# Turning the router's rows by DMA transposes instead of through PE in a fused attention and mixture-of-experts kernel

## The chip, the cores and the metric

The kernel runs on one core of one Trainium2 chip. The metric is the device time of the whole kernel in microseconds (us). Smaller is better. The core has five engines that run their own instruction streams and meet only at semaphores: PE (matrix products and transposes into PSUM), DVE, ACT and POOL (elementwise work), and SP, which here only issues DMAs.

## The reference

Two things are computed one after the other, for 2 batches of 768 positions:

```python
# attention with hash buckets, 16 heads (2 batches x 8) of 64 columns
scores = np.where(q_bucket == k_bucket, scale * q @ k.T, -1e9)
attn   = softmax(scores)
x      = attn @ v                       # (2, 768, 512), float32
# router
logits     = x @ w_gate                 # 8 experts
local_gate = sigmoid(x @ w_local)       # under 0.5: the fresh expert, else that of the position before
# experts, two layers with relu, one expert per position
out[s] = p[e] * (max(x[s] @ w1[e], 0) @ w2[e])
```

The router needs x transposed: the product over the 512 model columns wants those columns on the partitions.

## The kernel before

**Constants.** P = 128 partitions, NH = 16 heads, J = 6 row blocks of a batch, NC = 12 row blocks in all, DC = 4 column blocks of 128, NS = 48 attention steps (three per head: n = 3h + p). LEAD = 5 and LAG = 2 are how far scores run ahead and values behind.

**Attention.** Step n of PE's loop makes the transposed scores of step n (`scores_t`, L640 and L641), other preparation, and the values product of step n - 2 (`values`, L673 to L684). ACT takes exponentials (`exps`, L757) and their high half-precision part (`high`, L763). POOL subtracts to get the low part (`low`, L547); for the last two steps DVE does (`low_last`, L875). DVE normalises a finished head (`norm`, L881 to L891) and so writes two half-precision parts, high and low, of the head's 64 columns of x into XNS. Heads 0 to 7 are batch 0, heads 8 to 15 batch 1. A head's 64 columns are half a column block, so column block 3 of batch 1 is heads 14 and 15. Each engine's order is written out by hand: what stands earlier in an engine's loop runs earlier, and an instruction that waits holds all behind it on that engine.

**The router's rows.** For each of the 12 row blocks, `turn_rows` makes 8 PE transposes of 128 x 128 (two parts times four column blocks, L305) into a PSUM buffer `pG`, `copy_rows` copies the 128 x 1024 block to SBUF (`XTC`, L324 on DVE, L322 on ACT), and `logits` makes 12 small matmuls with 9 output columns (L313). Row blocks are numbered i. The six of batch 0 go i = 0 to 3 in steps 44 to 47 of the attention, i = 4 and 5 between and behind the last values. The six of batch 1, i = 6 to 11, come behind the last head (`rows_done(pe, NH - 1)`). ACT copies i = 4, 6, 8, 10, each behind half a piece of weight work; DVE the others.

**Behind the logits.** DVE waits for `s_gl` (all 12 row blocks) and for `s_rc` (small constants that POOL makes) and then runs a serial chain with PE that assigns positions to 19 tiles of 128 slots. It ends in the slot table (L1192 to L1194). POOL then gathers x rows by tile with indirect DMAs (`gather`, L1302), interleaved with the low parts of expert weights (`low_weights`, L407). ACT makes full scale and high parts of weights (`scale_weights`, L391; `high_weights`, L397; later L1446 and L1457) and issues weight loads (L1260). PE runs, per tile, `up` (24 matmuls, L1364; L1390 for the first tile) and `down` (24 matmuls, L1405). SP turns the gathered rows and the hidden rows with DMA transposes of 128 x 1024 half-precision elements (`turn_x`, L1276; `turn_h`, L1283).

**Queues.** SP issues in order: the max row of head 15 (`place_row`, L433) in step 43, then nothing until step 50, where it waits for the last head and issues the six x row stores of batch 1 (L518), two weight loads (L416), and, once `s_gl` and the stores have landed, eight quarter loads (L1260). POOL makes the small constants (L1042 to L1059) as soon as the last head is normalised, then `low_weights(6)`. The room in SBUF is shared by hand: XTC lay over the buffers T1 and T2; the four operand buffers OPS begin at CHUNK.

Of the kernel before, what the change touches and what calls it, by code (L numbers as in the profile page):

```python
# [6 lines left out]
def lsh_attention_moe_kernel(nc, q, k, v, proj, w_gate, w_local, w1, w2, x_rows, w_parts, out):  # L7
# [55 lines left out]
    with ctx:  # L63
# [67 lines left out]
        XTC = room[:, T_AT:T_AT + 3 * DM].bitcast(f16).rearrange("p (i a n) -> p i a n", i=3, a=2)  # L131
# [114 lines left out]
        s_wgp = sem("s_wgp")  # L246
        s_gt = sem("s_gt")
        s_gha = sem("s_gha")
        s_gc = sem("s_gc")
# [27 lines left out]
        pG = [o.bitcast(f16).rearrange("p (a n) -> p a n", a=2) for o in (pA[:, 0:512], pA[:, 512:1024], pB[:, 0:512])]  # L277
        pL = pA[:, 1024:1536]

        def logits_of(i):  # L280


            half = NC // 2
            if i < half:
                return i * B, i % 2, i - 1
            return (i - half) * B + 1, i % 3, i - 1 if i < half + 2 else 0 if i == half + 2 else i - 2

        def by_act(i):

            return i >= NS - TAIL and i % 2 == 0  # L290

        def copied(eng, i):

            if by_act(i):
                eng.wait_ge(s_gha, sum(by_act(k) for k in range(i + 1)))
            else:
                eng.wait_ge(s_gc, sum(not by_act(k) for k in range(i + 1)))

        def turn_rows(pe, i):
            c, buf, before = logits_of(i)  # L300
            if before > 0:
                copied(pe, before - 1)
            for a in range(2):
                for d in range(DC):
                    last = pe.transpose(pG[buf][:, a, d * P:(d + 1) * P], XNS[:, c, a, d * P:(d + 1) * P], idh[:, :])  # L305
            last.then_inc(s_gt, 1)

        def logits(pe, i):
            c, buf, _ = logits_of(i)
            copied(pe, i)  # L310
            for d in range(DC):
                for m, (a, r) in enumerate(((0, WGL), (1, WGH), (0, WGH))):
                    last = pe.matmul(pL[:, c * (E + 1):(c + 1) * (E + 1)], XTC[:, buf, a, d * P:(d + 1) * P], r[:, d, :],  # L313
                                     start=d == m == 0, stop=d == DC - 1 and m == 2)
            last.then_inc(s_gl, 1)

        def copy_rows(eng, i):
            _, buf, before = logits_of(i)
            eng.wait_ge(s_gt, i + 1)
            wait(eng, s_gl, before)  # L320
            if by_act(i):
                eng.activation(XTC[:, buf, :, :], pG[buf], ACT.Copy).then_inc(s_gha, 1)  # L322
            else:
                eng.tensor_copy(XTC[:, buf, :, :], pG[buf]).then_inc(s_gc, 1)  # L324


        TAIL = NS - LEAD + 1
# [124 lines left out]
        def _(sp):  # L452
# [118 lines left out]
        def _(pe):  # L571
# [133 lines left out]
            for n, h, p in steps():  # L705
# [14 lines left out]
                i = n - TAIL  # L720
                if pair(n - LAG) and n < NS:
                    values(n - LAG)
                    if 0 < i:
                        logits(pe, i - 1)
                    if 0 <= i:
                        if i == 0:
                            pe.wait_ge(s_wgp, 2)
                            pe.wait_ge(s_rmax, NS)
                            rows_done(pe, NH // B - 1)
                        turn_rows(pe, i)  # L730
                if p == 0 and fresh(h + 3):
                    turn_qk(h + 3, 0)

            values(NS - 2)
            turn_rows(pe, NS - TAIL)
            values(NS - 1)
            for i in range(NS - TAIL, NC // 2):
                logits(pe, i - 1)
                if i + 1 < NC // 2:
                    turn_rows(pe, i + 1)  # L740
# [791 lines left out]
```

## Time and profile before

| what | us |
|---|---|
| median of 3 runs | 486.23 |
| lowest and highest | 483.11, 488.06 |
| the profiled execution | 485.34 |
| its span on the core | 483.5 |
| PE busy | 455.8 |
| POOL busy | 340.0 |
| ACT busy | 302.1 |
| DVE busy | 262.5 |
| mean granted TensorE clock | 0.987 |

A time in the trace is counted from the start of the span. Busy is the sum of an engine's instructions. PE's matmuls are pipelined, so a busy PE is not yet one that nothing could make faster; the chain of work that ended last tells more. Between the span and the profiled execution's time lie 1.8 us.

### The profile page before, as it was taken

Reading aid. Unit: us, or ns where it says so; the run is one execution under the profiler, and the core shown is the slowest. Engines: PE = TensorE matmul, PEld = TensorE weight load, DVE = VectorE, ACT = ScalarE, POOL = GpSimd, SP = SyncE. Lnnn points to the kernel's source line nnn. Section 1 sums busy time; section 2 is a strip of 40 time slices with the busy share of each in tenths; the row PEclk is TensorE's granted clock in tenths of the full one; section 3 lists DMA queues with packets and bytes.
Section 4 is the critical chain, followed back from the end, with each engine's and each line's share of the span. In section 5 each row is a group of like instructions: output and inputs, shape, how many; then the busy total and the mean of one; then the engine's idle time right before and its main releaser. Section 6 shows DMA issues by size and latency. Waiting matters only on the chain.

```text
span 483.5 us, 11076 instructions
## 1 busy us (share of the span) xinstructions
PE 455.8 (94%) x4238; PEld 269.3 (56%) x4238; DVE 262.5 (54%) x385; ACT 302.1 (62%) x284; POOL 340.0 (70%) x193
## 2 busy tenths in 40 slices
PE   6699999999998999999977899999999999899994
PEld 3356777777666776767765344444444444344441
DVE  5676677666665666665475855344443344316331
ACT  2348988878888898887868145876566557600000
POOL 1226889897988798999824499999795847961101
PEclk9989999999999999999998899999999999999998
DMA  7745754566545833224009699999999999763440
GB/s 187 179 106 132 195 101 135 157 173 167 147 108 135 269 88 86 53 56 175 3 6 354 206 205 271 260 266 283 250 249 280 241 247 257 154 180 83 92 64 1
DMA packets 145284, 79.80 MB, mean 165 GB/s; under 512 B 90627, under 2 KB 136079, under 8 KB 145234
## 3 DMA queue, kind: packets, MB, share of 16 engines
q1 hardware_dynamic: 97726, 40.03, 38.1%
q10 hardware_dynamic: 44468, 30.93, 25.3%
q0 software_dynamic: 3040, 8.13, 5.5%
q8 instruction: 37, 0.61, 0.5%
q14 instruction: 13, 0.11, 0.1%
HBM read 47.99 MB, written 8.13 MB: 116 GB/s over the span
## 4 chain that ended last, share of the span: by engine, by line
PE 58%; ACT 13%; POOL 9%; ACTq 7%; DMA 4%; issue 3%; DVE 3%; SPq 1%; DVEq 0%
ACTq L1260 7%; ACT W L1457 7%; PE pA L623 6%; PE pB L641 6%; PE pA L624 6%; PE pB L640 6%; POOL W L407 6%; PE pO L1405 4%; PE pO L684 3%; PE pO L679 3%; PE pO L681 3%; PE pA L1364 3%; PE pP L1405 3%; POOL room L1302 3%; ACT room L1446 3%
## 5 line engine op out<-in xcount | busy, mean ns | idle before, releaser
L547 POOL TENSOR_TENSOR room<-room 128x1536 f16<-128x1536 f32 x46 | 142.5, 3106 | 39.0 <-ACT room L763 38.9
L407 POOL TENSOR_TENSOR W<-room,W 128x1024 f16<-128x1024 f32 x48 | 100.7, 2111 | 13.9 <-ACT W L1457 11.7
L854 DVE TENSOR_REDUCE room<-pA 128x2 f32<-128x1536 f32 x46 | 80.9, 1758 | 51.7 <-PE pA L624 51.7
L757 ACT ACTIVATE room<-pB 128x1536 f32<-128x1536 f32 x48 | 69.5, 1449 | 37.4 <-PE pB L641 36.1
L763 ACT ACTIVATE room<-room 128x1536 f16<-128x1536 f32 x48 | 71.2, 1484 | 1.5
L679 PE MATMUL pO<-W,room 128*128 128x64 f16 x576 | 62.0, 192 | 0.0
L684 PE MATMUL pO<-W,room 128*128 128x65 f16 x576 | 62.0, 194 | 0.0
L681 PE MATMUL pO<-W,room 128*128 128x65 f16 x576 | 61.9, 193 | 0.0
L640 PE MATMUL pB<-room 128*128 128x512 f16 x192 | 57.8, 326 | 0.4 <-ACT room L757 0.4
L641 PE MATMUL pB<-room 78*128 78x512 f16 x192 | 57.9, 326 | 0.0
L623 PE MATMUL pA<-room 128*128 128x512 f16 (+1 forms) x184 | 55.4, 326 | 1.5 <-DMA room<-room 1.4
L624 PE MATMUL pA<-room 76*128 76x512 f16 (+1 forms) x184 | 55.5, 326 | 0.0
L679 PEld LDWEIGHTS pO<-W,room 128*128 128x128 f16 x576 | 53.0, 98 | 2.3 <-issue 0.2
L681 PEld LDWEIGHTS pO<-W,room 128*128 128x128 f16 x576 | 52.9, 97 | 2.2
L1405 PE MATMUL pO<-W,room 128*128 x240 | 53.4, 379 | 0.0
L684 PEld LDWEIGHTS pO<-W,room 128*128 128x128 f16 x576 | 52.6, 97 | 0.0
L1309 POOL DMA_INDIRECT out<-room x19 | 18.9, 993 | 43.3 <-DVE room L1485 40.1
L1364 PE MATMUL pA<-W,room 128*128 x216 | 48.1, 379 | 1.3 <-POOL W L407 1.3
L1364 PE MATMUL pB<-W,room 128*128 x216 | 48.1, 379 | 0.6 <-DMA room<-room 0.6
L1405 PE MATMUL pP<-W,room 128*128 x216 | 48.1, 379 | 0.0
L1405 PEld LDWEIGHTS pO<-W,room 128*128 128x128 f16 x240 | 23.5, 98 | 28.3
L407 POOL TENSOR_TENSOR W<-XN,W 128x1024 f16<-128x1024 f32 x16 | 33.7, 2135 | 6.6 <-ACT W L1457 6.6
(219 smaller groups left out, 781.7 us busy)
## 6 DMA issues: line engine op xcount, KB each, us to landing
room<-in_moe_w ACTq DMA_DIRECT2D x44, 256.0 KB
room<-room SPq DMA_DIRECT2D x93, 96.0 KB, 2.2
W<-in_moe_w ACTq DMA_DIRECT2D x8, 1024.0 KB, 5.9
XN<-in_moe_w ACTq DMA_DIRECT2D x28, 256.0 KB
W<-in_moe_w SPq DMA_DIRECT2D x4, 1024.0 KB, 7.1
room<-in_q SPq DMA_DIRECT2D x16, 192.0 KB, 3.5
W<-in_v ACTq DMA_DIRECT2D x4, 768.0 KB, 6.3
x_rows<-XN SPq DMA_DIRECT2D x12, 256.0 KB, 3.2
```

What stands on the lines that cost most here:

```text
L407: pool.tensor_tensor(parts(r)[:, 1, cols], scaled(r)[:, cols], parts(r)[:, 0, cols], ALU.subtract).then_inc(lows(r, half)[0], 1)
L547: pool.tensor_tensor(PTL[:, n % NP, :, :], E32[:, n % 2, :, :], PTH[:, n % NP, :, :], ALU.subtract).then_inc(s_lo, 1)
L623: pe.matmul(o, QA[:, b, cols], KA[:, b, n0:n1], start=True, stop=False)
L624: last = pe.matmul(o, QB[0:R_S, b, cols], KB[0:R_S, b, n0:n1], start=False, stop=True)
L640: pe.matmul(o, KA[:, b, cols], QA[:, b, n0:n1], start=True, stop=False)
L641: last = pe.matmul(o, KB[0:R_ST, b, cols], QB[0:R_ST, b, n0:n1], start=False, stop=True)
L679: pe.matmul(o, PTH[:, n % NP, i, cols], VL[g // HG][:, g % HG, j, :], start=False, stop=False, skip_group_check=True)
L681: pe.matmul(o1, PTL[:, n % NP, i, cols], VH[g // HG][:, g % HG, j, 0:D + 1], start=False, stop=False, skip_group_check=True)
L684: last = pe.matmul(o1, PTH[:, n % NP, i, cols], VH[g // HG][:, g % HG, j, 0:D + 1], start=False, stop=j == J - 1, skip_group_check=True)
L854: dve.reduce_max(RM[:, g % 2, 2 * p:2 * p + 2], scores_in(n)[:, :].rearrange("p (i s) -> p i s", i=2), AX.X).then_inc(s_rmax, 1)
L1364: last = pe.matmul(o, l[:, cols], r, start=k == m == 0, stop=k == n - 1 and m == 2)
L1405: last = pe.matmul(pY[t % 2][:, 0:DM], HT[:, t % 2, a, f * P:(f + 1) * P], W[:, bass.ds(at + low * CHUNK, 512)], start=a == f == 0 and low ...
```

## The change

The six row blocks of batch 0 are turned by six DMA transposes of 128 x 1024 elements each, issued by SP in step 43, into a buffer of their own. Column blocks 0 to 2 of batch 1 are turned by twelve DMA transposes of 128 x 384 elements (six row blocks, two parts), issued by SP in step 45. PE makes the logits of batch 0 two row blocks at a time in steps 46 and 47 and the last two behind the last values, then the part of batch 1's logits that comes from column blocks 0 to 2. Behind the last head only column block 3 of batch 1 goes through PE: 12 transposes in two groups of six, one copy of 128 x 768 on DVE, one on ACT, and 18 matmuls. ACT does all four pieces of weight 6 first and the copy after them. POOL does `low_weights(6)` ahead of the small constants instead of behind them. ACT's first half of `scale_weights(7)` moves behind the exponential of the logits.

```diff
+        XTC = [room[:, at:at + J * DM].bitcast(f16).rearrange("p (i a n) -> p i a n", i=J, a=2) for at in (CHUNK, T_AT)]
...
+        pG = [pA[:, k * 512:(k + 1) * 512].bitcast(f16)[:, 0:J * P] for k in range(2)]
...
+        def logits(pe, b, i, blocks):
+            c = i * B + b
+            for d in blocks:
                 for m, (a, r) in enumerate(((0, WGL), (1, WGH), (0, WGH))):
+                    last = pe.matmul(pL[:, c * (E + 1):(c + 1) * (E + 1)], XTC[b][:, i, a, d * P:(d + 1) * P], r[:, d, :],
+                                     start=c == d == m == 0, stop=d == DC - 1 and m == 2, skip_group_check=True)
+            return last
+        TURNS = (NS - LEAD, NS - LEAD + 2)
...
+                if n == TURNS[0]:
+                    sp.wait_ge(s_ST, PAIRS * (NH - 2))
+                    sp.wait_ge(s_PV, PAIRS * (NH - 3) + 1)
+                    rows_done(sp, H - 1)
+                    for i in range(J):
+                        sp.dma_start_transpose(XTC[0][:, i, :, :].rearrange("p a (d n) -> p (a d) n", n=P),
+                                               XNS[:, i * B, :, :].rearrange("p a n -> p (a n)")).then_inc(s_xt_in[0], 16)
+                if n == TURNS[1]:
+                    sp.wait_ge(s_qkt, 2 * NH)
+                    sp.wait_ge(s_hash, 2 * NH)
+                    for g in (NH - 2, NH - 1):
+                        sp.wait_ge(s_asm[g % NQ], 96 * (g // NQ + 1))
+                    rows_done(sp, NH - 3)
+                    for i in range(J):
+                        for a in range(2):
+                            sp.dma_start_transpose(
+                                XTC[1][:, i, a, 0:(DC - 1) * P].rearrange("p (d n) -> p d n", n=P),
+                                XNS[:, i * B + 1, a, 0:(DC - 1) * P]).then_inc(s_xt_in[1], 16)
...
                 if pair(n - LAG) and n < NS:
                     values(n - LAG)
-                    if 0 < i:
-                        logits(pe, i - 1)
-                    if 0 <= i:
...
-                        turn_rows(pe, i)
+                i = B * (n - TURNS[0] - 3)
+                if 0 <= i < J and n < NS:
+                    if i == 0:
+                        pe.wait_ge(s_wgp, 2)
+                        pe.wait_ge(s_rmax, NS)
+                        rows_turned(pe, 0)
+                    for k in range(i, i + B):
+                        logits(pe, 0, k, range(DC)).then_inc(s_gl, 1)
...
             values(NS - 2)
-            turn_rows(pe, NS - TAIL)
             values(NS - 1)
...
+            for k in range(B * (NS - TURNS[0] - 3), J):
+                logits(pe, 0, k, range(DC)).then_inc(s_gl, 1)
+            rows_turned(pe, 1)
+            for i in range(J):
+                logits(pe, 1, i, range(DC - 1))
+            rows_done(pe, NH - 1)
+            for k in range(2):
+                for i in range(HJ):
+                    for a in range(2):
+                        at = (2 * i + a) * P
+                        last = pe.transpose(pG[k][:, at:at + P], XNS[:, (k * HJ + i) * B + 1, a, (DC - 1) * P:DC * P], idh[:, :])
+                last.then_inc(s_gt, 1)
+            for k in range(2):
+                pe.wait_ge(s_gc[k], 1)
+                for i in range(k * HJ, (k + 1) * HJ):
+                    logits(pe, 1, i, range(DC - 1, DC)).then_inc(s_gl, 1)
...
             norm(NH - 1)
-            for i in range(NS - TAIL, NC // 2):
-                if not by_act(i):
-                    copy_rows(dve, i)
+            dve.wait_ge(s_gt, 1)
+            dve.tensor_copy(last_rows_in(0), pG[0].rearrange("p (k n) -> p k n", n=P)).then_inc(s_gc[0], 1)
...
         def _(pool):
+            low_weights(pool, EARLY, 0)
+            low_weights(pool, EARLY, 1)
             pool.wait_ge(s_x, NH)
...
-            low_weights(pool, EARLY, 0)
-            low_weights(pool, EARLY, 1)
...
             for piece in (scale_weights, high_weights):
                 for half in range(2):
                     piece(act, EARLY, half)
-                    copy_rows(act, next(rows))
+            act.wait_ge(s_gt, 2)
+            act.activation(last_rows_in(1), pG[1].rearrange("p (k n) -> p k n", n=P), ACT.Copy).then_inc(s_gc[1], 1)
+            act.wait_ge(s_dl, 1)
+            act.activation(EX[:, :, :], DL[:, :, :], ACT.Exp, scale=1.0 / (XS * WS)).then_inc(s_ex, 1)
             act.wait_ge(s_PV, NS - LAG)
             scale_weights(act, EARLY + 1, 0)
...
         def _(pe):
-            rows_done(pe, NH - 1)
-            for i in range(NC // 2, NC):
-                turn_rows(pe, i)
-                if i > NC // 2 + 1:
-                    logits(pe, i - 2)
-            logits(pe, NC - 2)
-            logits(pe, NC - 1)
```

## Rows read from the trace of the kernel before

**Rows 1.** The chain in order of time: start us, us, what.

```profile
260.10 0.27 DVE room L1138
...
271.26 1.15 POOL room L1302
...
410.12 4.24 POOL W L407 x2
414.49 5.35 PE pA L1364 x24
```

**Rows 2.** Stretches: us, busy us of PE, PEld, DVE, ACT, POOL, granted clock, DMA share, GB/s.

```profile
260.00:272.00 12.00, 9.65 (x64) 4.22 (x63) 10.08 (x50) 7.25 (x9) 1.46 (x2) 0.72 0.85 315
283.00:414.00 131.00, 129.72 (x600) 58.64 (x600) 61.30 (x56) 87.82 (x88) 109.56 (x62) 1.00 1.23 260
```

**Rows 3.** PE's longest waits from 270 on: us in total, times, longest.

```profile
PE pA L1364 <- POOL W L407: 1.3, 1, 1.3
```

**Rows 4.** DVE's timeline: start us, us, engine, line, form [idle before <-releaser].

```profile
247.46 1.76 DVE L875 TENSOR_TENSOR room<-room 128x1536 f16<-128x1536 f32 x1 [0.62 <-ACT room L763]
250.64 0.17 DVE L881 TENSOR_SCALAR DEN<-pO 128x6 f32<-128x6 f32 x1 [0.82 <-PE pO L684]
252.26 0.56 DVE L891 TENSOR_TENSOR XN<-pO,XN 128x384 f16<-128x384 f32 x1
258.33 0.69 DVE L324 COPY room<-pB 128x1024 f16<-128x1024 f16 x1 [1.17 <-PE pB L305]
```

**Rows 5.** PE's timeline around step 47 and behind the last head.

```profile
242.95 0.38 PE L640 MATMUL pB<-room 128*128 128x512 f16 x1
254.68 0.61 PE L305 MATMUL pB<-idh,XN 128*128 128x128 f16 x8
265.66 4.53 PE L1091 MATMUL pP<-W,idh 128*128 128x512 f16 x12
```

**Rows 6.** PE's logits in the chain that ended last: start us, us, what.

```profile
259.23 0.77 PE pA L313 x24
```

**Rows 7.** ACT's timeline.

```profile
244.47 1.45 ACT L757 ACTIVATE room<-pB 128x1536 f32<-128x1536 f32 x1 [0.19 <-PE pB L641]
247.34 1.04 ACT L391 ACTIVATE room<-W 128x1024 f32<-128x1024 f32 x1
258.15 1.02 ACT L322 ACTIVATE room<-pA 128x1024 f16<-128x1024 f16 x1
262.26 2.00 ACT L397 ACTIVATE W<-room 128x1024 f16<-128x1024 f32 x2
```

**Rows 8.** POOL's timeline.

```profile
252.91 0.20 POOL L1042 TENSOR_SCALAR room<-col_id 128x8 f32<-128x8 f32 x1 [8.59 <-DVE XN L891]
253.78 0.10 POOL L1052 MEMSET room<- 128x2 f32 x1
256.49 4.23 POOL L407 TENSOR_TENSOR W<-room,W 128x1024 f16<-128x1024 f32 x2 [1.81 <-ACT W L397]
```

**Rows 9.** SP's issues, timeline: start us, us, what (a group with several: their sum).

```profile
231.89 1.41 SPq L433 DMA_DIRECT2D room<-room  x2
252.90 3.24 SPq L518 DMA_DIRECT2D x_rows<-XN  x6
276.61 7.22 SPq L1276 DMA_TRANSPOSE room<-room  x3
419.92 1.23 SPq L1276 DMA_TRANSPOSE room<-room  x1
456.20 2.61 SPq L1283 DMA_TRANSPOSE room<-XN  x2
```

**Rows 10.** DMA from 419 to 424 us, 40 slices of 0.125: busy tenths, GB/s.

```profile
DMA  0000000000000000189999999982000000000000
GB/s 0 0 0 0 0 0 0 0 0 0 0 0 0 0 0 0 23 172 231 211 221 213 209 197 215 203 167 37 0 0 0 0 0 0 0 0 0 0 0 0
```

**Rows 11.** Busy by stretch over the last steps of attention, columns as in rows 2.

```profile
233.40:242.80 9.40, 8.93 (x188) 7.35 (x187) 2.91 (x7) 8.16 (x7) 8.13 (x4) 1.00 0.02 4
```

More of the change, by code:

```diff
@@ L246, in lsh_attention_moe_kernel @@
         s_wgp = sem("s_wgp")
+        s_xt_in = [sem(f"s_xt_in{b}") for b in range(B)]
         s_gt = sem("s_gt")
-        s_gha = sem("s_gha")
-        s_gc = sem("s_gc")
+        s_gc = [sem(f"s_gc{k}") for k in range(2)]
         s_gl = sem("s_gl")
@@ L275, in prep_in @@
             return pO if g < AHEAD and half == 1 else pP
-        pG = [o.bitcast(f16).rearrange("p (a n) -> p a n", a=2) for o in (pA[:, 0:512], pA[:, 512:1024], pB[:, 0:512])]
+        pG = [pA[:, k * 512:(k + 1) * 512].bitcast(f16)[:, 0:J * P] for k in range(2)]
         pL = pA[:, 1024:1536]
[L280 to L311, printed above, removed]
-                for m, (a, r) in enumerate(((0, WGL), (1, WGH), (0, WGH))):
[L313 to L324, printed above, removed]
@@ L329, in lsh_attention_moe_kernel, with last_rows_in @@
+        def last_rows_in(k):
+            return XTC[1][:, k * HJ:(k + 1) * HJ, :, (DC - 1) * P:DC * P].rearrange("p i a n -> p (i a) n")
+        TURNS = (NS - LEAD, NS - LEAD + 2)
         LAST = NS - 2
@@ L937, in _ @@
                     low_last(n)
-                i = n - TAIL
-                if 0 <= i < NS - TAIL:
-                    if i == 0:
-                        dve.wait_ge(s_asm[(NH - 1) % NQ], 96 * ((NH - 1) // NQ + 1))
-                        dve.wait_ge(s_asm[(NH - 2) % NQ], 96 * ((NH - 2) // NQ + 1))
-                    copy_rows(dve, i)
             norm(NH - 1)
-            for i in range(NS - TAIL, NC // 2):
-                if not by_act(i):
-                    copy_rows(dve, i)
+            dve.wait_ge(s_gt, 1)
+            dve.tensor_copy(last_rows_in(0), pG[0].rearrange("p (k n) -> p k n", n=P)).then_inc(s_gc[0], 1)
         pS, pR = pO, pB[:, 512:1024]
@@ L1060, in _ @@
                       allow_small_or_imprecise_dtypes=True).then_inc(s_rc, 1)
-            low_weights(pool, EARLY, 0)
-            low_weights(pool, EARLY, 1)
         @block.scalar
         def _(act):
-            rows = filter(by_act, range(NC))
             for piece in (scale_weights, high_weights):
@@ L1127, in _ @@
             ch = Chain(dve, s_rt)
-            for i in range(NC // 2, NC):
-                if not by_act(i):
-                    copy_rows(dve, i)
             dve.wait_ge(s_rc, 9)
```

15 lines of the change are left out of this document (2 added, 13 removed).

## The prediction, made before the changed kernel ran

> **What bounds the kernel now.** I read the chain that ended last first, in order of time. Through the router it is one serial thread: PE's logits, DVE's first reduction at 260.10 and, 11.16 us later, POOL's first gather at 271.26 [rows 1]. From there POOL, ACT and the load issues carry it to 410, and PE alone to the end. The stretches say more: from 283 to 414 PE is busy for 129.7 of 131 us [rows 2], and its longest wait for weights after 270 is 1.3 us [rows 3]. So behind 271 two streams are both nearly full, PE and POOL with ACT. Both start from the same slot table. If the table comes earlier, both start earlier, and the end moves with them. If one of them had a fixed start, the end would not move. I see none: the weight loads that fill the DMA engines are issued by ACT behind POOL's work.
>
> Then I read the timelines of each engine from 230 to 272. Behind the last head (norm(15) ends at 252.82) DVE waits another 7.3 us for the logits [rows 1, 4]. PE, DVE and ACT pass six row blocks of batch 1 round: 8 transposes, a copy of 0.69 or 1.02 us, 12 matmuls [rows 4, 5, 7]. ACT is the slow member, since a weight piece of 1.0 us stands between its copies. Over the last steps of attention the DMA engines are idle: share 0.02 from 233.4 to 242.8 [rows 11].
>
> **What goes.** 84 of 96 PE transposes, 10 of 12 large copies, and six trips PE, copy, PE behind the last head.
>
> **What comes on SP, batch 0.** SP is free after the max row of head 15, at 231.89 + 1.41 = 233.3 [rows 9]; the semaphores it then waits for belong to step 41 and are long there. One DMA transpose of 128 x 1024 takes 1.23 us to issue, two in a row 2.61, so 1.31 each [rows 9]. Issued alone at 419.92, its data moves from 421.0 to 422.5 at 200 to 215 GB/s [rows 10], so it has landed about 2.55 us after its start. The sixth starts at 233.4 + 5 x 1.31 = 239.95 and lands at 242.5.
>
> PE wants them in step 46, before scores_t(47), which began at 242.95 [rows 5]. Ahead of it now stand 24 logits: 0.77 us [rows 6], 0.6 without the tail that overlaps. So 242.35 is the landing at which nothing is lost. What is queued behind this wait is scores_t(47), then exps(47) at 244.47 [rows 7], low_last(47) at 247.46 and values(47), which ends at 250.64 [rows 4]: all of it sets the end of attention. Against that, steps 44 and 45 lose a turn of 8 transposes ahead of each scores_t, 0.45 us that comes back if the rows have landed. Bounds: attention ends 0.6 us earlier (rows landed) to 0.5 later (1.37 us an issue). I take 0.3 later, since the landing is what PE meets last: norm(15) ends at 253.1.
>
> Here a rule of the Trainium skill can be weighed. The row shows 200 to 215 GB/s for a transpose that is alone [rows 10]. The Trainium skill, Advanced Engine Details and Errata, section X-Bar Transpose (TRN2), says that transpose DMAs are as fast as regular ones, 350 to 400 GB/s. By that the sixth would land some 0.6 us earlier and PE would not wait; the trace does not agree, and I go by the trace.
>
> **Batch 1, column blocks 0 to 2.** SP starts them at 233.4 + 6 x 1.31 = 241.2. No row shows a 128 x 384 transpose. Lower bound: three eighths of 1.23, 0.46. Upper bound: the full 1.27. Plain issues cost 3.24 / 6 = 0.54 whatever they carry [rows 9]; taking 0.4 to 0.54 as fixed and three eighths of the rest gives 0.71 to 0.80. I take 0.77: issues end at 250.4, landing about 1.0 later at 251.4. PE asks at 250.9 + 0.6 for the last two blocks of batch 0, so 251.5: hidden, by attention itself. The 54 matmuls take 54 x 0.026 = 1.4 us, to 252.9, still before norm(15). SP reaches the x stores before the last head is done, so nothing queued behind (stores, weight loads) is late.
>
> **Behind the last head.** Transposes from 253.1: 8 take 0.61 with their tail [rows 5], six 0.5, twelve 0.8. DVE's copy of 128 x 768: 0.55; ACT's 0.8, from 253.9 to 254.75, both three quarters of the variable part of the large copies [rows 4, 7]. Nine matmuls 0.35. Logits complete: **255.1**.
>
> **The POOL move.** DVE also waits for nine small constants. Before, they took 252.91 to 253.88, hidden [rows 8]. Now low_weights(6) stands ahead. ACT starts weight 6 at 247.34 + 0.3 = 247.65, four pieces at 1.0 [rows 7]; the first high half is done at 250.7. POOL: 250.75 + 4.23 = 255.0, constants 0.97 [rows 8]: **256.0**. So the constants and not the logits release DVE, 0.9 us after them. What is moved past is nothing that anyone waited for; without the cover of the logits the move costs this 0.9. Bounds 255.7 to 256.5.
>
> **The router's serial part** stays 11.16 us. It contains 12 idle matmuls of PE in 4.53 us at a granted clock of mostly half (0.72 over the stretch) [rows 2, 5]. At half throughout (1.2 GHz) they would take 12 x 0.43 = 5.1. PE has less work ahead of them now. I add 0.2, bounds 0 to 0.6. The first gather meets the tail of weight loads, which still run to about 270: 0.1, bounds 0 to 0.8.
>
> **Sum.** 260.10 - 256.0 = 4.1 earlier, less 0.2 and 0.1: 3.8. Against the profiled execution (485.34; span 483.5 and 1.8 around it) 481.5; against the median shown, 486.23, which is 0.9 above it, **482.4**. With the bounds together the gain is 2.2 to 5.1: 481.1 to 484.0 on the median. The single runs of before spread by 2.5 us either way, so I widen this case's own range to 479.5 to 485.
>
> **Rivals.**
> - A: the small transposes cost as much to issue as the large. SP ends at 241.2 + 12 x 1.27 = 256.4, landing 257.4, PE's 54 matmuls 258.8, then 2.0: 260.8, 0.7 later than before. The stores start 3.5 us later and the loads behind them meet the gathers: 0.5. **487.4**. For it: nothing shows that the cost follows size; plain DMAs don't. Against: 1.23 beside 0.54 says that most of it follows blocks. It starts to cost at 0.87 each and eats the gain at 1.21. Chance 0.13.
> - B, the other side: six in a row back up, as three did at 276.61 in 7.22 us, 2.4 each [rows 9]. The sixth lands at 233.4 + 12 + 2.55 = 248.0, 5.6 past the point that costs nothing; PE stands in step 46 with scores_t(47) behind it. At half of that for each small one, SP ends at 262.2, logits at 262.2 + 1.0 + 1.4 + 2.0 = 266.6, 6.5 later: **492.7**. It decides from 1.86 us an issue. Against: those three stood among gathers, while here the DMA share is 0.02 [rows 11]. Chance 0.1.
> - C: the table is earlier, but PE or the weight stream is held by something else, and most of the gain comes back as PE waits before 414: **485.5**. Against: PE's 1.3 us of waiting says that the streams are balanced, for: balanced streams leave little to hide a shift in one. Chance 0.1.
> - D: batch 0's rows are there when PE asks; attention ends 0.6 earlier instead of 0.3 later: **481.5**. Chance 0.08. The rule of the Trainium skill named above would bring this about; the trace's rate speaks against it.
> - E: the clock stays at its lower level through all idle matmuls and the gathers lose 0.8 to the loads: 1.1 less gain, **483.5**. Chance 0.04.
> - The forecast: 0.55.
>
> **How the numbers follow.** 1% either way, about what can be told from no change, is 481.4 and 491.1. The forecast lies 0.8% below, so its better side is over the line: about 0.25 for faster, with D. Slower is B and a bad form of A, 0.12. The rest, 0.63, within 1%. The range takes in the forecast, D, E, C and A: 479.5 to 488; outside are B and what is better than all sums.
>
> **What would show it.** SP: six transposes from 233.3 to about 241.2, twelve to about 250.4; over 252.8 means A. PE: a wait in step 46 for a DMA of 0.1 to 1 us; over 3 means B. DVE's wait for the first reduction ends by POOL's constants, at 256.0. First gather near 267.5. From 283 on PE is as full as before; waits for POOL or a DMA there over 3 us mean C. I am wrong in kind if the rows' path still ends later than 258, or if the gather moves by over 3 us and the end does not.

## The result, and the profile after

The changed kernel is slower, by 1.3%. It took 492.99 us, the median of 4 runs (489.37 to 496.86), against 485.36 us for the kernel before, the median of 4 (483.11 to 488.06): a ratio of 1.0127, 95% interval 1.0068 to 1.0187. The prediction was 482.4 us, 0.8% faster. Here and below a ratio compares undisturbed executions alone, and one more than 1.5% above the fastest of its kernel is left out of it, while medians and means over all runs take in every execution. The profiled execution of the changed kernel took 489.37 us, its span is 487.6 us.

The attention's last heads don't start at the same time in any two traces: the first DVE instruction of norm(13), long before any changed instruction matters, lies at 232.46 in the trace of before and at 227.34 in this one, and a second trace of the kernel before has it at 228.06. So I call that instruction the mark and count from it.

| us behind the mark | before | after | forecast |
|---|---|---|---|
| SP has issued batch 0's six transposes | – | 10.04 | 8.7 |
| SP has issued batch 1's twelve | – | 27.4 | 17.9 |
| last head normalised (norm(15) ends) | 20.36 | 24.82 | 20.6 |
| first reduction on the logits | 27.64 | 32.85 | 23.5 |
| first gather starts | 38.79 | 44.12 | 35.0 |

The slot table, on which everything behind depends, comes 5.3 us later instead of 3.8 us earlier. First SP's issues in the changed kernel (start us, us, queue, line, form), which answer to [rows 9]:

```profile
226.77 1.41 SPq L407 DMA_DIRECT2D room<-room  x2
228.29 9.09 SPq L481 DMA_TRANSPOSE room<-XN  x6
237.62 17.11 SPq L492 DMA_TRANSPOSE room<-XN  x12
254.83 3.28 SPq L512 DMA_DIRECT2D x_rows<-XN  x6
```

The six large ones take 9.09 / 6 = 1.52 us each. The twelve, each with three eighths of the data, take 17.11 / 12 = 1.43 each. The same two groups once more, now with the shortest, median and longest issue in ns, and with the time from issue to landing:

```profile
L481 SPq DMA_TRANSPOSE room<-XN x6: 1329/1356/1998, 228.3 to 235.9; - x6
DMA to landing us min/median/max: 3.4/4.2/5.0
L492 SPq DMA_TRANSPOSE room<-XN x12: 1248/1257/2161, 237.6 to 253.5; - x12
DMA to landing us min/median/max: 2.3/2.4/4.4
```

Then PE's timeline (start us, us, line, form [idle before <-releaser]), to be read beside [rows 5]:

```profile
240.40 0.17 PE L292 MATMUL pA<-WGL,room 128*128 128x9 f16 x1 [3.71 <-DMA room<-XN]
...
241.03 0.59 PE L634 MATMUL pB<-room 128*128 128x512 f16 x1
...
243.12 0.63 PE L635 MATMUL pB<-room 78*128 78x512 f16 x1
...
255.88 0.19 PE L292 MATMUL pA<-WGL,room 128*128 128x9 f16 x1 [5.35 <-DMA room<-XN]
```

PE stands twice, 3.71 us in step 46 for batch 0's rows and 5.35 us for batch 1's, with 24 and 54 small matmuls behind. Between them stands something that I had not priced: the same 128 x 512 matmul of scores_t(47) that took 0.38 us before [rows 5] takes 0.59 here. The stretches say why. Columns as in [rows 2]: the granted clock, the DMA share and GB/s are the last three.

```profile
239.00:240.00 1.00, 0.00 (x0) 0.00 (x0) 1.00 (x1) 0.00 (x0) 0.00 (x0) 0.54 0.97 213
242.00:243.00 1.00, 1.00 (x6) 0.60 (x4) 0.00 (x0) 0.00 (x0) 0.00 (x0) 0.50 0.48 98
260.00:272.00 12.00, 10.54 (x67) 4.27 (x64) 9.91 (x49) 8.07 (x9) 0.54 (x1) 0.59 0.98 355
283.00:414.00 131.00, 126.67 (x582) 56.92 (x579) 57.65 (x53) 84.79 (x85) 106.10 (x61) 0.99 1.20 253
```

At the end of its wait PE is granted 0.54, and behind it 0.50, the lower of its two levels, 1.2 GHz. exps(47), which ACT makes of scores_t(47), started 12.0 us behind the mark before (244.47 in [rows 7]) and starts 16.5 behind it now:

```profile
243.79 1.45 ACT L761 ACTIVATE room<-pB 128x1536 f32<-128x1536 f32 x1 [5.20 <-PE pB L635]
```

Behind the last head DVE waits for PE and not for POOL's constants, and the serial part of the router is what it was. DVE's timeline:

```profile
251.60 0.56 DVE L895 TENSOR_TENSOR XN<-pO,XN 128x384 f16<-128x384 f32 x1
258.17 0.56 DVE L944 COPY room<-pA 128x768 f16<-128x768 f16 x1 [6.02 <-PE pA L740]
260.19 0.26 DVE L1123 TENSOR_REDUCE room<-pA 128x12 f32<-128x96 f32 x1 [1.46 <-PE pA L292]
```

POOL's:

```profile
254.98 0.10 POOL L1051 MEMSET room<- 128x2 f32 x1
...
271.46 1.16 POOL L1287 DMA_INDIRECT room<-x_rows,room  x1 [15.58 <-DVE room L1179]
```

POOL's last constants are written at about 255, five us before DVE starts. From 260.19 to 271.46 lie 11.27 us, where it was 11.16 [rows 1]. In the stretch from 283 to 414 PE is busy for 126.67 us, 3.05 less than in [rows 2]; PE's longest wait for POOL was 1.3 us [rows 3], just behind that stretch, and is now 4.3, inside it (us in total, times, longest):

```profile
PE pA L1349 <- POOL W L381: 4.3, 1, 4.3
```

The sum of the two traces: the part before the mark is 5.1 us shorter (chance), the part from mark to gather is 5.3 longer, the part from gather to end is 216.1 against 212.3, 3.9 longer: 4.1 in all, 487.6 against 483.5. The last part, too, varies without any change: it is 224.3 us in the second trace of the kernel before, an execution of 493.49 us. So one trace tells surely only what happened between mark and gather. What that is worth in time had to come from many timed runs.

### The profile page after: what moved, and what is told of

Same layout as the page of the kernel before. It is cut to its first block, busy times and chain, and to the rows that moved or that the text cites. A ratio compares the mean times of both kernels' runs of the same rounds, so it can differ in the third digit from the quotient of the medians.

```text
span 487.6 us, 10910 instructions
## 1 busy us (share of the span) xinstructions
PE 455.0 (93%) x4154; PEld 266.6 (55%) x4154; DVE 258.0 (53%) x378; ACT 298.5 (61%) x281; POOL 339.9 (70%) x193
## 4 chain that ended last, share of the span: by engine, by line
PE 62%; POOL 12%; ACT 8%; ACTq 6%; SPq 5%; issue 3%; DVE 2%; DMA 1%; DVEq 0%
POOL W L381 8%; PE pA L617 6%; PE pA L618 6%; PE pB L634 6%; PE pB L635 6%; ACTq L1245 5%; PE pO L1390 5%; PE pA L1349 5%; ACT W L1442 4%; PE pP L1390 4%; POOL room L1287 3%; PE pB L1349 3%; SPq L492 3%; PE pO L678 3%; PE pO L675 3%; PE pO L673 3%
## 5 line engine op out<-in xcount | busy, mean ns | idle before, releaser
L678 PE MATMUL pO<-W,room 128*128 128x65 f16 x576 | 62.8, 195 | 0.0
L675 PE MATMUL pO<-W,room 128*128 128x65 f16 x576 | 62.8, 194 | 0.0
L1349 PE MATMUL pA<-W,room 128*128 x216 | 49.7, 388 | 4.3 <-POOL W L381 4.3
L1390 PEld LDWEIGHTS pO<-W,room 128*128 128x128 f16 x240 | 23.5, 98 | 28.3
## 6 DMA issues: line engine op xcount, KB each, us to landing
room<-in_moe_w ACTq DMA_DIRECT2D x44, 256.0 KB
XN<-in_moe_w ACTq DMA_DIRECT2D x28, 256.0 KB
x_rows<-XN SPq DMA_DIRECT2D x12, 256.0 KB, 3.2
```

The lines of the kernel that those rows point to most:

```text
L675: pe.matmul(o1, PTL[:, n % NP, i, cols], VH[g // HG][:, g % HG, j, 0:D + 1], start=False, stop=False, skip_group_check=True)
L678: last = pe.matmul(o1, PTH[:, n % NP, i, cols], VH[g // HG][:, g % HG, j, 0:D + 1], start=False, stop=j == J - 1, skip_group_check=True)
L1349: last = pe.matmul(o, l[:, cols], r, start=k == m == 0, stop=k == n - 1 and m == 2)
L1390: last = pe.matmul(pY[t % 2][:, 0:DM], HT[:, t % 2, a, f * P:(f + 1) * P], W[:, bass.ds(at + low * CHUNK, 512)], start=a == f == 0 and low ...
```

## The experiments

All kernels below are either the changed kernel or the kernel before with one edit. "Table" is the start of the first gather behind the mark; it was 38.79 before and 44.12 after. A ratio is always to the kernel before, timed in the same rounds.

**The changed kernel and the kernel before, once more.**

> The changed kernel once more, unaltered, for a second trace. Times are counted from a mark: the start of norm(13)'s first DVE instruction (232.46 before, 227.34 in the first trace after). If the loss sits in the waits for the transposes, this trace repeats them: PE waits about 5 us in step 46 for batch 0's rows, the last head is normalised 24.8 us behind the mark (20.4 before), the logits are complete at 32.8 (27.6 before) and the first gather at 44.1 (38.8 before). If the 4.3 us wait of PE for weights at 392 and the earlier start of the attention by 5.1 us are chance of one execution, they differ here; if they belong to the change, both come again.

Measured: 494.95 us, ratio 1.0173 (1.0121 to 1.0226). Last head at 24.05, first reduction 32.81, table 44.07, each within 0.8 us of the first trace. PE stands 3.0 us for batch 0's rows and 6.1 for batch 1's. (The 5 us that the expectation names belong to batch 1's wait; the one in step 46 was 3.7.) The mark lies at 231.29 here, and PE's wait of 4.3 us for POOL is not there: both of these were chance of one execution. So the places behind the mark can be compared between traces, and the loss is real.

> The kernel before, unaltered, for a second trace: it tells how much of the times by stage is chance. From the mark on the router should repeat within 0.2 us (last head 20.4, logits 27.6, first gather 38.8). The place of the mark (232.5 in the first trace) and the length of the part behind the first gather (212.3) are what I expect to differ, each by up to 5 us. The ratio should be 1.00.

Measured: 487.82 us, ratio 0.9998 (0.9947 to 1.0048). Last head 20.36, first reduction 28.13, table 39.38: 0.0, 0.5 and 0.6 from the first trace. A move of the table under 0.6 us is noise here; the part behind it moved by 12 us (224.3 against 212.3) with nothing changed, in an execution that took 493.49 us against 485.34.

> The changed kernel, unaltered, on the same chip and in the same rounds as the delayed one. From the mark on it should repeat: last head 24.1 to 24.8, logits 32.8, first gather 44.1. Ratio 1.013 to 1.017. If it exceeds the delayed kernel's ratio by more than the intervals, the change costs something behind the table too.

Measured: the ratio is 1.0068 (1.0004 to 1.0132), from only 4 of the 13 runs. Over all runs the mean is 494.3 us (13) against 488.6 us (29), 5.7 us or 1.2% more. Last head 24.68, table 44.23 again. The three ratios of the changed kernel are 1.0127, 1.0173 and 1.0068; I read the loss as 1 to 1.5%.

**Batch 0's logits behind the last head's values, so that nobody stands in step 46.**

```
-  if 0 <= i < J and n < NS:
-      if i == 0:
-          pe.wait_ge(s_wgp, 2)
-          pe.wait_ge(s_rmax, NS)
-          rows_turned(pe, 0)
-      for k in range(i, i + B):
-          logits(pe, 0, k, range(DC)).then_inc(s_gl, 1)
...
   values(NS - 1)
+  pe.wait_ge(s_wgp, 2)
+  pe.wait_ge(s_rmax, NS)
+  rows_turned(pe, 0)
+  for k in range(J):
+      logits(pe, 0, k, range(DC)).then_inc(s_gl, 1)
```

> The changed kernel with all of batch 0's logits behind the last values, so that PE waits for no transpose inside the attention. If the wait in step 46 is the whole loss of the router, the last head comes back to 20.4 us behind the mark and the first gather to about 39.7. If SP's issues are the bound (26.4 us for the 18 transposes, from 0.9 behind the mark to 27.3), the attention comes back but the logits are complete only at about 31.8 and the first gather is at about 43, some 1 us better than with the change; the time then stays over that of before.

Measured: ratio 1.0151 (1.01 to 1.0203), 493.4 us. The last head is normalised at 19.84, half a us earlier than before the change, so the whole 4.5 us that attention lost are gone. But the first reduction is at 32.53 and the table at 43.78: only 0.3 us of it arrive. PE has one wait instead of two (us in total, times, longest):

```profile
PE pA L292 <- DMA room<-XN: 8.8, 1, 8.8
```

So the wait in step 46, with what follows from it, is real and costs attention 4.5 us, and it doesn't set the table. What PE now waits for are the rows of batch 1 behind it.

**Only batch 1's small transposes, and 8 us earlier.** They go out in step 43; batch 0 goes through PE, two thirds of it in steps 44 to 47 as before.

```
-  TURNS = (NS - LEAD, NS - LEAD + 2)
+  TURNS = (NS - LEAD,)
...
-                    for i in range(J):
-                        sp.dma_start_transpose(XTC[0][:, i, :, :].rearrange("p a (d n) -> p (a d) n", n=P),
-                                               XNS[:, i * B, :, :].rearrange("p a n -> p (a n)")).then_inc(s_xt_in[0], 16)
...
+                    else:
+                        logits_0(pe, i - 1)
+                    turn_rows(pe, i)
```

> Only batch 1's column blocks 0 to 2 by DMA (12 transposes, 128 x 384), issued in step 43; batch 0 through PE in the attention's last steps as before, and POOL's constants ahead of its weight piece as before. If SP's issue time of 1.43 us for each transpose is what matters, SP is done 19.4 us behind the mark, the rows have landed at about 21, the logits are complete at 24.6 to 25.5 and the first gather is at about 36.5, 2 to 3 us ahead of before. If the end follows the slot table, the kernel is 2 to 3 us faster than before (ratio 0.994 to 0.996). If the weight stream behind 283 us has its own pace, the ratio is 1.00.

Measured: ratio 0.9945 (0.9874 to 1.0016), 489.09 us. The twelve take as long with nothing in front of them (SP's timeline, then PE's):

```profile
230.70 18.64 SPq L510 DMA_TRANSPOSE room<-XN  x12
...
252.00 0.19 PE L294 MATMUL pA<-WGL,room 128*128 128x9 f16 x1 [3.10 <-DMA room<-XN]
```

That is 1.55 us each. The last one still lands 23.6 us behind the mark (252.00 - 228.44), 3.1 us after PE wants it. The table is at 39.14, as before the change: what the shorter tail gains, this wait takes. The time isn't told from that of before.

**The price by size.** Batch 0 as twelve of 128 x 512, batch 1 as twelve of 128 x 256 and twelve of 128 x 128, on the kernel with the late logits.

```
+                        for a in range(2):
+                            sp.dma_start_transpose(XTC[0][:, i, a, :].rearrange("p (d n) -> p d n", n=P),
+                                                   XNS[:, i * B, a, :]).then_inc(s_xt_in[0], 16)
...
+                                XTC[1][:, i, a, 0:2 * P].rearrange("p (d n) -> p d n", n=P),
+                                XNS[:, i * B + 1, a, 0:2 * P]).then_inc(s_xt_in[1], 16)
...
+                                XTC[1][:, i, a, 2 * P:3 * P].rearrange("p (d n) -> p d n", n=P),
+                                XNS[:, i * B + 1, a, 2 * P:3 * P]).then_inc(s_xt_in[1], 16)
```

> What one DMA transpose costs to issue, by its size. As the run with late logits, but batch 0 in 12 transposes of 128 x 512 and batch 1 in 12 of 128 x 256 and 12 of 128 x 128. Seen so far: 128 x 1024 in a row of six 1.5 us, 128 x 384 in a row of twelve 1.38 to 1.55. If the cost follows the size, these take about 0.9, 0.6 and 0.5 us. If it is one price for each instruction, all three take 1.4, and SP is done only 51 us behind its start. If 384 is dear because it is no power of two, 512 and 256 are cheap and 384 is the exception.

Measured, in one run: 510.29 us. SP's issues:

```profile
232.01 17.08 SPq L482 DMA_TRANSPOSE room<-XN  x12
249.33 15.73 SPq L493 DMA_TRANSPOSE room<-XN  x12
265.10 15.26 SPq L498 DMA_TRANSPOSE room<-XN  x12
```

| columns | us each, group / count | median of one issue |
|---|---|---|
| 1024 | 1.52 | 1.36 |
| 512 | 1.42 | 1.27 |
| 384 | 1.43 | 1.26 |
| 256 | 1.31 | 1.25 |
| 128 | 1.27 | 1.23 |

The rows for 1024 and 384 are those of the changed kernel; in the other traces a group of 1024 took 1.49 to 1.56 us each and one of 384 1.38 to 1.55. An eighth of the data costs 84% of the time. The price is one of the instruction, with at most 0.25 us in it that goes with the size. By the medians it is 0.12; single issues of about 2 us lift the means of the larger ones. The sizes ran in one order only, and the last group ran while PE, DVE, ACT and POOL stood idle, so some of the small difference may come from the place and not from the size.

**The small transposes taken away, the large ones kept.** All of batch 1 goes through PE behind the last head, with three buffers and the copies shared by ACT and DVE.

```
-                            sp.dma_start_transpose(
-                                XTC[1][:, i, a, 0:(DC - 1) * P].rearrange("p (d n) -> p d n", n=P),
-                                XNS[:, i * B + 1, a, 0:(DC - 1) * P]).then_inc(s_xt_in[1], 16)
...
+            for i in range(J):
+                turn_rows(pe, i)
+                if i > 1:
+                    logits_1(pe, i - 2)
```

> The other half alone: batch 0 by six DMA transposes in step 43, its logits behind the last values; all six row blocks of batch 1 through PE behind the last head as before, three copies on ACT (now behind all four weight pieces) and three on DVE. SP needs 9.2 us and is done 10 us behind the mark, landing at 12.7; nobody waits for that. If only a wait of PE in the attention or a full SP queue costs, the last head is at 19.8 (20.4 before, since steps 44 and 45 lost their turns) and the logits at 25 to 26 (27.6 before). If transposes in flight slow other work by themselves, the last head is later than 20.4. Ratio 0.995 to 1.00.

> The run with batch 0 alone by DMA and late logits once more, for its time: it brought the first gather to 36.5 us behind the mark (38.8 before) and a ratio of 0.9995 with an interval of 0.994 to 1.005. If an earlier table moves the end as much as a later one did (5.5 us later cost 4.3 to 5.0 us), the ratio is 0.995 to 0.997. If the weight stream behind the table keeps its own pace, it is 1.00 and PE waits 3 to 5 us for weights as in the first trace.

Measured (the same kernel twice, on two chips): last head 19.86 and 19.85, first reduction 25.50 and 26.45, table 36.51 and 37.46; ratios 0.9995 (0.9937 to 1.0052) and 0.9998 (0.9952 to 1.0043), 485.92 and 486.58 us. Against the kernel with the late logits, from which it differs by the small transposes and what replaces them, the table is 7.3 and 6.3 us earlier. Here PE turns 48 blocks behind the last head where it turned 12, and is still sooner done than twelve issues. This is the test of the cause: with the twelve gone, the table's delay and the loss are gone. And nothing is left of the wait for batch 0: its six transposes are out by 237.33, 9.9 us before the last head is normalised (247.26), and PE's list of waits has none for them. SP's timeline:

```profile
228.35 8.98 SPq L503 DMA_TRANSPOSE room<-XN  x6
...
247.33 3.10 SPq L522 DMA_DIRECT2D x_rows<-XN  x6
```

A table that is 2.3 or 1.3 us earlier than before the change gives no time that could be measured. The intervals are too wide to settle it, though: a gain passed on in full would be 0.9953 and 0.9973, inside both. In the first of the two traces PE stands for POOL in the stretch before 414:

```profile
PE pA L1347 <- POOL W L403: 4.4, 1, 4.4
```

In the second it stands there too, 3.6 us at most. But the same wait of 4.3 us was in the first trace of the changed kernel, whose table is late, so it doesn't go with an early table.

**The clock behind the wait.** The changed kernel with sixteen idle matmuls in step 46, ahead of PE's wait.

```
   if i == 0:
       pe.wait_ge(s_wgp, 2)
       pe.wait_ge(s_rmax, NS)
+      for _ in range(16):
+          pe.matmul(pP[:, 0:512], idh[:, :], parts(0)[:, 0, 0:512], start=True, stop=True)
       rows_turned(pe, 0)
```

> The changed kernel with 16 idle matmuls of PE (128 x 512, 3.5 us) ahead of its wait for batch 0's rows in step 46. In the first trace PE waited 3.7 us there, then made scores_t(47) at a granted clock of 0.50 in 3.0 us instead of 1.5, and the last head was 4.5 us late. If the lower clock is part of the loss, scores_t(47) takes 1.5 us again at a granted clock of 1.0 and the last head is at 22.3 to 23 behind the mark instead of 24.1 to 24.8. If only the wait counts, the last head stays at 24 to 25. The slot table is set by the second set of transposes and stays at 44.

Measured, in one run: 494.69 us. PE does them instead of standing, is granted 1.00 behind them and makes scores_t(47) at full speed:

```profile
240.56 3.62 PE L722 MATMUL pP<-W,idh 128*128 128x512 f16 x16
...
244.74 0.38 PE L634 MATMUL pB<-room 128*128 128x512 f16 x1
...
245.83 0.38 PE L635 MATMUL pB<-room 78*128 78x512 f16 x1
```

The last head is at 23.23, against 24.05, 24.68 and 24.82 in three traces of the changed kernel. The clock's part can be told better from PE's first logits of batch 0 on, since the landing itself varies (12.3 to 13.1 behind the mark). From there to the end of norm(15) it is 11.7 to 11.8 us in those three traces and 10.5 here (244.12 to 254.61). So about 1.3 of the 4.5 us that attention loses are the clock. The rest is the wait: scores_t(47) starts 3.2 us later than before (13.7 against 10.5 behind the mark). scores_t(47) itself took 2.7 us in the first trace, not the 3.0 of the expectation. The table is at 43.91: no gain, since batch 1's rows set it.

**A later table by itself.** The kernel before, with the router's first reduction done 15 or 19 times.

```
-  ch.link(dve.reduce_max(M1[:, :], l8, AX.X))
+  for _ in range(15):
+      ch.link(dve.reduce_max(M1[:, :], l8, AX.X))
```

> The kernel before, with 14 repeats of DVE's first reduction behind the logits (0.29 us each, 4.1 us in all), so that only the slot table comes later. If the end follows the slot table one for one, this costs 4.1 us, ratio 1.008. If the weight stream hides it or has its own pace, it costs under 1.5 us. If a shift upsets the balance of PE and the weight stream, it costs over 6.

> The kernel before with 18 repeats of DVE's first reduction, so that the slot table is 5.3 us late, as late as with the change, and nothing else differs: no transposes in the attention, x stores and weight loads where they were. If the late table is the whole loss, this kernel has the ratio of the changed one (1.013 to 1.017). If the change loses something more behind the table, this one has 1.008 to 1.011 and the changed one more than that.

DVE's timeline, in the first of the two and in the second:

```profile
257.96 4.34 DVE L1139 TENSOR_REDUCE room<-pA 128x12 f32<-128x96 f32 x15 [1.08 <-PE pA L313]
```

```profile
256.62 5.51 DVE L1139 TENSOR_REDUCE room<-pA 128x12 f32<-128x96 f32 x19 [0.62 <-PE pA L313]
```

Measured: with 15, the table is at 42.99, 4.2 us later, and the ratio 1.0063 (0.9999 to 1.0126), 490.03 us. With 19 it is at 44.29, 5.5 us later, and the ratio 1.0169 (1.0115 to 1.0222), 492.39 us; the mean of its 6 runs is 492.9 against 488.6. The second kernel has the changed kernel's table, to 0.2 us, and nothing else of the change, and it is as slow: 492.39 against 492.99 us, a ratio of 1.0169 against 1.0127, 1.0173 and 1.0068. So the later table alone gives the loss, within what could be measured. The means over all runs in the same rounds, 492.9 and 494.3, differ by 1.4 us, which is inside their scatter; whether a us or two comes from elsewhere isn't settled.

**An earlier table.** From the kernel with the small ones early: only eight of them (row blocks 0 to 3), so that they land in time, the other two row blocks by PE and ACT.

```
+  BY_DMA = 4
...
-                    for i in range(J):
+                    for i in range(BY_DMA):
                         for a in range(2):
...
+            for i in range(BY_DMA, J):
+                turn_front(pe, i)
...
+            for i in range(BY_DMA, J):
+                copy_front(act, i)
```

> As the run with batch 1 alone by DMA, but only row blocks 0 to 3 of it by DMA (8 transposes instead of 12). Column blocks 0 to 2 of row blocks 4 and 5 go through PE behind the last values, under the normalisation of the last head, and are copied by ACT. If the twelve issues in a row were what kept the table from coming earlier (rows landed 23.5 us behind the mark, 3.1 us after PE asked), 8 land at about 17.5, the logits are complete at 22.8 behind the mark (27.6 before, 27.9 with twelve) and the first gather is at 34. If the path behind the last head costs more than I think (copies, cold PE), the logits come at 24 to 25. If the end follows the table, the kernel is 4 to 5 us faster than before, ratio 0.990; if the weight stream has its own pace, 1.00.

Measured: ratio 1.0017 (0.9969 to 1.0065). The first reduction is at 24.07, 3.6 us earlier than before the change, and the table still at 38.80. Nearly all of the 3.6 us goes in two places of DVE (L1176 and L1177), both while POOL does low_weights(6). Of the pair at L1176 the first instruction took 1.71 us. DVE's timeline:

```profile
251.72 0.26 DVE L1170 TENSOR_REDUCE room<-pA 128x12 f32<-128x96 f32 x1 [1.24 <-PE pA L294]
...
252.62 1.79 DVE L1176 SCALAR_TENSOR_TENSOR room<-room 128x12 f32<-128x12 f32 x2
254.33 2.19 DVE L1177 SCALAR_TENSOR_TENSOR room<-room 128x96 f32<-128x96 f32 x1
```

POOL's:

```profile
252.18 4.22 POOL L421 TENSOR_TENSOR W<-room,W 128x1024 f16<-128x1024 f32 x2 [2.30 <-ACT W L411]
```

In the kernel before POOL does this at the same place, 24.0 us behind the mark, and ends at 256.49 + 4.23 = 260.72 [rows 8]. That is just ahead of the two instructions, so nothing stood. DVE's timeline before:

```profile
261.00 0.25 DVE L1144 SCALAR_TENSOR_TENSOR room<-room 128x12 f32<-128x12 f32 x2
```

Earlier logits run into it.

In the next kernel POOL does low_weights(6) ahead of its constants, as in the changed kernel, DVE copies row blocks 4 and 5 of batch 0, ACT does its four weight pieces first, and PE's turns stand ahead of the last values.

```
+  low_weights(pool, EARLY, 0)
+  low_weights(pool, EARLY, 1)
   pool.wait_ge(s_x, NH)
...
-  low_weights(pool, EARLY, 0)
-  low_weights(pool, EARLY, 1)
...
+  copy_rows(dve, 4)
+  copy_rows(dve, 5)
   norm(NH - 1)
```

> In the run with 8 transposes the logits came 24.1 us behind the mark (27.6 before), but two DVE instructions of 0.25 us (both operands in SBUF) took 1.8 and 2.2 us while POOL's low_weights(6) ran, and the first gather was at 38.8 as before. Here low_weights(6) stands ahead of POOL's constants, as in the change, ACT does all of weight 6 first, DVE copies batch 0's last two blocks ahead of norm(15), and the PE turns stand ahead of the last values. If POOL held DVE up, the two instructions are 0.25 us again, the first reduction is at 23 to 23.5 (POOL's constants set it) and the first gather at 34.3 to 35, 4 us ahead of before. If it was PE's half clock or something else, the serial part stays 14 us long. If the end follows the table, the ratio is 0.992; if the weight stream has its own pace, 1.00.

DVE's timeline in this kernel:

```profile
253.49 0.26 DVE L1167 TENSOR_REDUCE room<-pA 128x12 f32<-128x96 f32 x1 [1.13 <-PE pA L294]
...
254.40 0.25 DVE L1173 SCALAR_TENSOR_TENSOR room<-room 128x12 f32<-128x12 f32 x2
254.56 0.25 DVE L1174 SCALAR_TENSOR_TENSOR room<-room 128x96 f32<-128x96 f32 x1
```

Measured: the same two forms take 0.25 us now. The first reduction is at 24.37 though the last head is 1.6 us later (22.01), the table at 35.62, 3.2 us earlier than before the change and 8.5 earlier than after it. The ratio is 1.0026 (0.9986 to 1.0066), 487.01 us. In its trace PE is busy for all 131.00 us from 283 to 414, the part behind the gather is 212.6 us (212.3 before), and the span is 477.3, the shortest of all: in this one execution the earlier table passed to the end in full. The timed runs don't bear that out. A gain of 3.2 us would be a ratio of 0.9934, and the interval excludes it. But this kernel differs from the one before in much more than the place of its table, so what swallowed the gain isn't shown.

**SP's later loads by themselves.** The kernel before, with SP's eight quarter loads held until the router's first scan is done.

```
+  sp.wait_ge(s_loc, 1)
```

> The kernel before with one wait more on SP: the eight quarter loads of weights 12 and 13 start once the router's first scan is done, 2.2 us later, as late as with the change (262.2 against 260.0). The slot table doesn't move. With the change the span behind the first gather was 216.1 us, 212.3 before, and PE waited 4.3 us for weights. If the later loads upset the stream of weights, this kernel loses 2 to 4 us behind the first gather, ratio 1.004 to 1.008. If that loss was chance, or comes from somewhere else, the ratio is 1.00.

Measured: ratio 1.0006 (0.9971 to 1.0042), with the loads 2.4 us later behind the mark (257.74 - 227.76 against 260.02 - 232.46). They may be that late against the table at no cost. The x stores, which the change moved from 20.4 to 27.5 us behind the mark, were not delayed by themselves in any run.

## Why the prediction failed, point by point

**The small transposes' price: the step that failed.** The prediction took 0.77 us for a 128 x 384, between "three eighths of 1.23" and 1.27. It measured 1.43. The interpolation treated 0.4 to 0.54 us as fixed, from plain issues, and the rest as going with the columns. (That plain issues cost 0.54 whatever they carry is more than [rows 9] show: 0.54 for an x store and 0.70 for a max row.) The run over sizes shows the reverse: about 1.27 is the fixed part and the columns are worth 0.25 at most. So the twelve took 17.1 us and not 9.2, and SP was done 27.4 us behind the mark and not 17.9: 7.9 of these 9.5 us are this one term, 1.3 the six large ones. For the large ones the prediction took 1.31, the mean of two; six in a row took 1.52, so the bound of 1.37 was under it, too.

**The landing.** 2.55 us behind the start were taken from a transpose that was alone [rows 10]. Six in a row needed 3.4 to 5.0, and PE could go on 13.1 us behind the mark (240.40) where 10.0 was forecast: 1.0 of that since the sixth was issued later, 2.0 from the landing (235.88 to 240.40 is 4.5). PE was to wait a fraction of a us and stood 3.7. What stood behind the wait was named rightly: scores_t(47) starts 3.2 us later, and exps(47), the last values and norm(15) about 4.5, since the clock adds to the wait.

**The rate of a transpose.** Six in a row moved 151 GB/s at a DMA share of 0.91, under the 200 to 215 of one alone. The Trainium skill, Advanced Engine Details and Errata, section X-Bar Transpose (TRN2), expects 350 to 400 GB/s. The trace does not agree, and the gap is wider than the prediction had it.

**The clock.** No term stood for it ahead of the last head. By the end of a wait of 3.7 us PE was at the lower level, and scores_t(47) took 2.7 us instead of 1.5. The run with idle matmuls shows that this is worth about 1.3 us.

**Behind the last head.** Rival A had the mechanism of this part right: SP's issues set the logits. It let SP end at 256.4, 23.9 behind the mark, and the logits come 0.7 later than before. They came 5.2 later: 3.6 of the 4.5 us between are the landing of batch 1's rows (28.5 behind the mark against 24.9), and 0.9 lie behind it, where A had 1.4 + 2.0 us to the first reduction and it measured 4.3. The late attention has no share in it beyond 0.3 us, as the run with the late logits shows. POOL's constants, which were to release DVE at 256.0, were done before the logits, so the move on POOL cost nothing. It can do more than that: where the logits came early, low_weights(6) behind the constants held DVE up by 3.5 us, and ahead of them it didn't (1.79 and 2.19 us against 0.25 and 0.25). I had put the move down as a pure cost. The router's serial part was right: 11.27 against 11.16 + 0.2.

**From the table to the end.** The prediction let a gain in the table pass fully. No kernel's timed runs showed such a gain: tables 1.3, 2.3 and 3.2 us earlier gave 0.9998, 0.9995 and 1.0026. Only the last excludes a gain passed on in full, and that kernel has other changes beside it. The result is what rival C, with its chance of 0.1, would give. A later table does pass: 5.5 us gave 1.7% (8 us by the ratio, 5.0 by the medians and 4.3 by the means over all runs). That 4.2 us gave 0.6% (0 to 1.3) fits less well, but excludes neither. So a delay passes, and a gain was not seen to; that the price of the table is one-sided around the kernel before is likely, not shown, since no run moved the table earlier by itself. Nor is rival C's mechanism shown, that the gain comes back as PE's waits before 414. PE's longest wait for POOL was 1.3 us before [rows 3], 4.4 and 3.6 in the traces with the table 2.3 and 1.3 us earlier, but none in the one with the table 3.2 us earlier, and 3.4 with the table 5.5 us later. The reason stays open.

**Range and chances.** The time lies above the range's end of 488.0, and "slower" had 0.12. Of the rivals A was nearest in kind. Its time, 487.4, was short because its price, taken as an upper bound, was below the true one. Rival B's place, PE standing in step 46, was right as well, with a smaller price than its 5.6 us. That B's 492.7 is nearly the measured median is luck: it took 2.4 us for a large transpose and 1.2 for a small one, where 1.52 and 1.43 were measured. Three of the signs named beforehand were seen, in times behind the mark: SP ended later than A's limit (27.4 against 20.3), PE stood over 3 us in step 46, and the rows' path ended later than 258 (32.9 against 25.5). The two were priced as if only one of them could be true, though both hang on one number, what a DMA transpose costs in a row; I treated the cheap case of both as likely without a row for either.

## What to carry to other kernels

Here a DMA transpose of 128 x 128 to 128 x 1024 elements cost its queue 1.3 to 1.5 us whatever it carried, so few large ones in time cost nothing and many small ones did: cut the count, not the bytes. Put such an issue ahead by its price times its number plus the landing in a row, not the landing of a single one, and keep PE's wait for it where nobody stands behind it. Before counting on a gain from a serial part, delay it by a few us in the kernel as it is, and take even that as half an answer: here a delay passed to the end, and none of the three kernels with an earlier table was measurably faster.

## What the runs showed of the hardware

- The issue price above: 1.27 us at 128 columns, 1.52 at 1024. At 384 columns the DMA engines are not what limits: during the twelve of 384 columns their share was 0.57, at 74 GB/s, against 0.91 and 151 GB/s during the six of 1024.
- A DVE instruction with both operands in SBUF stood while POOL worked on a tensor_tensor with both operands in SBUF: 1.79 and 2.19 us instead of 0.25, each ending 0.12 us behind one of POOL's two (252.18 + 2.11 = 254.29, and 256.40), while DVE's instruction with one operand in PSUM, inside the same stretch (252.33, 0.26 us), did not stand. The Trainium skill, SBUF — State Buffer, section Who interferes with whom, states it so: a DVE instruction with two SBUF inputs contends with a GpSimd instruction that reads SBUF. The trace agrees; in the kernel with POOL's work moved (and three other edits) the 3.5 us were back.
- A PE wait of 3.7 us was followed by 2.7 us of work, at a granted clock of 0.50, that takes 1.5 at 1.00.
